# Adding the epsilon of the softmax sum with another VectorE instruction, and moving the embedding scaling into the attention loop

## The reference

```python
scores = scale * q @ k.T + bias           # 2 batches, 8 heads, 768 positions, head_dim 64
scores = where(is_global | is_local, scores, -1e9)
a = exp(scores - max(scores))
a = a / (sum(a) + 1e-9)                   # the 1e-9 is what the change is about
x = (a @ v), rows gathered to [1536, 512]
# first mixture: top-1 of 8 experts by cosine with normalised embeddings
en = emb / (norm(emb) + 1e-6)
x = gate * relu(x[mask] @ w1[e]) @ w2[e]
# second mixture: all 4 experts, weighted by given probabilities
out = sum_e p[:, e] * relu(x @ w1[e]) @ w2[e]
```

## Time and profile before

| | us |
|---|---|
| median of 3 runs | 911.2 |
| lowest, highest | 910.04, 911.38 |
| the profiled execution, whole | 910.04 |
| its span, first to last instruction | 908.2 |

### The profile page before, as it was taken

One profiled execution on the slowest core, in us unless ns is written; L12 is line 12 of the kernel. 1 busy time (PEld: TensorE's weight loads), 2 busy tenths in 40 slices (PEclk: granted clock), 3 DMA queues, 4 the chain that ended last, 5 costly groups with the idle time before them and its releaser, 6 DMA issues.

```text
span 908.2 us, 12900 instructions
## 1 busy us (share of the span) xinstructions
PE 860.9 (95%) x4433; PEld 695.1 (77%) x4434; DVE 300.3 (33%) x776; ACT 221.3 (24%) x476; POOL 288.8 (32%) x162
## 2 busy tenths in 40 slices
PE   7999945999999999999999999999999999999998
PEld 5666623788888788788888888888888888888886
DVE  6777770444444443223121212121212121211212
ACT  4878750033333323311111111111111111111010
POOL 4462613057777778630000650000830001400000
PEclk9999976999999999999999999999999999999999
DMA  6899623146666667620000230000320000001001
GB/s 246 265 315 342 221 78 140 31 124 213 205 204 205 195 220 220 174 94 1 1 0 0 70 116 0 0 0 0 115 71 0 0 0 0 1 0 46 29 17 46
DMA packets 33075, 90.96 MB, mean 100 GB/s; under 512 B 4232, under 2 KB 4616, under 8 KB 33040
## 3 DMA queue, kind: packets, MB, share of 16 engines
q1 hardware_dynamic: 23056, 54.86, 18.1%
q10 hardware_dynamic: 8064, 29.36, 10.6%
q0 software_dynamic: 1920, 6.29, 2.2%
HBM read 72.67 MB, written 17.83 MB: 100 GB/s over the span
## 4 chain that ended last, share of the span: by engine, by line
PE 84%; DMA 8%; DVE 3%; issue 2%; POOL 2%; SPq 1%; ACT 1%; DVEq 0%; ACTq 0%
PE ps L1209 29%; PE ps L1196 29%; PE ps L1153 10%; PE ps L1135 7%; DMA win<-qkv 3%; DMA xg<-x_sorted 3%; PE ps L1008 2%; PE ps L1034 2%; PE ps L1020 2%; POOL x_sorted L473 1%; PE ps L1143 1%; PE ps L1125 1%; PE ps L979 1%; PE ps L1048 1%; ACT arena L528 1%
## 5 line engine op out<-in xcount | busy, mean ns | idle before, releaser
L1209 PE MATMUL ps<-ring,h 128*128 128x512 f32 x1152 | 275.9, 390 | 0.0
L1196 PE MATMUL ps<-ring 128*128 (+1 forms) x864 | 256.4, 389 | 0.0
L278 POOL TENSOR_TENSOR ring<-raw,ring 128x1024 fp32r<-128x1024 f32 x96 | 227.9, 2403 | 84.0 <-ACT ring L273 81.1
L1209 PEld LDWEIGHTS ps<-ring,h 128*128 128x128 f32 x1152 | 215.6, 188 | 44.6
L1196 PEld LDWEIGHTS ps<-ring 128*128 128x128 f32 x864 | 162.1, 188 | 34.0 <-DVE x2b L940 0.2
L947 DVE SCALAR_TENSOR_TENSOR h<-ps,h 128x512 fp32r<-128x512 f32 x96 | 66.3, 691 | 366.3 <-ACT h L597 366.3
L597 ACT ACTIVATE h<-ps 128x512 fp32r<-128x512 f32 x96 | 57.6, 600 | 427.3 <-PE ps L1196 427.3
L273 POOL CAST ring<-raw 128x1024 fp32r<-128x1024 f32 x36 | 38.0, 1055 | 374.8 <-PE ps L1196 320.3
L1196 PE MATMUL ps<-x2b,ring 128*128 (+1 forms) x288 | 112.0, 389 | 0.0
L273 ACT CAST ring<-raw 128x1024 fp32r<-128x1024 f32 x60 | 62.2, 1051 | 176.9 <-PE ps L1153 116.7
L1135 PE MATMUL ps<-ring,xT 128*128 x384 | 91.8, 395 | 0.6 <-DVE xT L900 0.6
(11 more groups left out here) (116 smaller groups left out, 490.2 us busy)
## 6 DMA issues: line engine op xcount, KB each, us to landing
raw<-wts ACTq DMA_DIRECT2D x56, 512.0 KB, 4.2
raw<-wts SPq DMA_DIRECT2D x40, 512.0 KB, 3.8
win<-qkv SPq DMA_DIRECT2D x32, 320.0 KB, 4.1
x_sorted<-ring SPq DMA_DIRECT2D x20, 256.0 KB, 4.9
xg<-x_sorted SPq DMA_DIRECT2D x17, 256.0 KB, 3.4
y_sorted<-yrow SPq DMA_DIRECT2D x16, 256.0 KB, 4.0
win<-qkv SPq DMA_DIRECT2D x8, 384.0 KB, 6.3
result<-xrow SPq DMA_DIRECT2D x12, 256.0 KB, 2.1
```

Of the source, the lines that this page charges most:

```text
L278: nc.gpsimd.tensor_tensor(w_part(u, 1)[:, q * CW:q * CW + CW], raw[:, q, :], w_part(u, 0)[:, q * CW:q * CW + CW].bitcast(F32), ALU.subtrac ...
L1196: ins = nc.tensor.matmul(ps[:, 4 + f % 2, :], w_part(u1, wp)[:, k * F + f * P:k * F + f * P + P], x2T(xp, k)[:, bass.ds(g * 512, 512)], st ...
L1209: ins = nc.tensor.matmul(ps[:, t, :], h2[:, f % 2, hp_, t * P:t * P + P], w_part(u1 + 1, wp)[:, f * DM:f * DM + DM], start=(f == 0 and n = ...
```

## The change

1. `sums` loses its last axis and is [128, 12, 2]. The memset of the constant 1e-9 goes. ScalarE's accumulator writes the same values to the new places.
2. `denominators` is a `tensor_scalar` that adds the immediate 1e-9 to 2 values per partition, where it was a `tensor_reduce` from 4 values to 2. It stands at the same place in the pipeline, 48 times.
3. `scale_embeddings` is no longer called ahead of the bias table. It is run beside the first pair of heads after step 1 (the other branch, which these inputs do not take, calls it at its start).
4. The unused tensor `spare` (160 bytes per partition) goes. With the smaller `sums` all tensors after it lie 256 bytes lower, and `den`, `inv` and `nmax` 96 bytes lower.

```diff
-        sums = sb("sums", [P, DUO, 2, 2])
+        sums = sb("sums", [P, DUO, 2])
...
-        sb("spare", [P, 40])
...
-                                                   accum_out=sums[:, i, hh, 0:1])
+                                                   accum_out=sums[:, i, hh:hh + 1])
...
-            nc.vector.memset(sums[:, :, :, 1], 1e-9)
...
-            scale_embeddings()
...
-                    nc.vector.tensor_reduce(den[:, i % 2, :], sums[:, i, :, :], AX.X, ALU.add).then_inc(denom_ready, 1)
+                    nc.vector.tensor_scalar(den[:, i % 2, :], sums[:, i, :], 1e-9, None, ALU.add).then_inc(denom_ready, 1)
...
-                         {3: keep_embeddings, 6: expert_weights}, {squares: 5})
+                         {1: scale_embeddings, 3: keep_embeddings, 6: expert_weights}, {squares: 5})
```

More of the change, by code:

```diff
@@ L650, in _, with scale_embeddings @@
             dve.wait_ge(bias_built, 1)
+            def scale_embeddings():
+                dve.wait_ge(emb_root, 1)
+                step(nc.vector.tensor_scalar(norm_e[:, 2:3], norm_e[:, 1:2], 1e-6, None, ALU.add))
+                step(nc.vector.reciprocal(norm_e[:, 3:4], norm_e[:, 2:3]))
+                nc.vector.tensor_scalar(embn_t, emb_t, norm_e[:, 3:4], None, ALU.mult).then_inc(emb_scaled, 1)
+                nc.vector.memset(lg[:, :, :, :], 0.0)
+                step(nc.vector.memset(turner[:, :, P:], 0.0))
             def keep_embeddings(idle_times=2):
@@ L750, in _ @@
                                (normalise, 4)],
-                         {3: keep_embeddings, 6: expert_weights}, {squares: 5})
+                         {1: scale_embeddings, 3: keep_embeddings, 6: expert_weights}, {squares: 5})
             with dve.Else():
                 done[0] = before_paths
+                scale_embeddings()
                 keep_embeddings(1)
```

## The result

| | before, us | after, us |
|---|---|---|
| median (4 runs each, same chip) | 911.29 | 922.96 |
| lowest, highest | 910.04, 911.38 | 920.11, 924.50 |
| span of the profiled execution | 908.2 | 920.3 |

A forecast was written before the change was run, and what follows sets the result against it. TensorE was taken to bound attention, with 0.67 us of slack per step. Holds of 3.7 + 3 + 3.8 = 10.5 us on the profiled 910.04 gave 920.5, forecast as 921, range 910.5 to 928.

The forecast's parts named there:

- What bounds the kernel: Attention: TensorE sets the 2.06 us step almost without idle time; VectorE delays up to 0.67 us are hidden.
- Part 1: Embedding scaling moved behind step 1: frees nothing ahead of the bias table and fits a 1.83 us VectorE hole; cost 0.
- the embeddings miss their hole: Rival at attention's start: the multiplication slips, stands until GpSimd's subtraction ends, 1 to 2 us more; inside the forecast's case.
- start: Attention from 12.66 to 26.53 us: denominators held by GpSimd's first four quarters, 3.7 us lost after slack.
- Part 2: Dropped memset and tensors moved by 256 bytes: 0, with 0.5 us to both sides for the addresses.
- Part 3: The 48 new tensor_scalar instructions in attention: each waits for the end of GpSimd's current instruction; 10.5 us in all.
- L732's or L713's: Bounds for the new instruction: never held like the reciprocal, 0 us, or held like the SBUF tensor_scalar; the second was taken.
- middle, eight quarters: Attention's eight single GpSimd quarters: holds partly recovered from TensorE's window waits, 3 us, bounds 1 and 6.
- last four quarters: Attention from 97.75 to 112.35 us: one step per GpSimd quarter, square held again, 3.8 us, bounds 1 and 6.
- Two values take no second port: Rival: the new instruction is never held, like the reciprocal; 911 us, not slower; chance 0.20.
- Held, but hidden: Rival: waits fall into slack and window waits, only attention's start pays; 2 to 5 us, 913 to 916; chance 0.12.
- Faster: Rival: a gain from shorter undisturbed instructions, at most 0.8 us, or an earlier bias table; chance 0.02.

The follow-up runs named there:

- e5: The kernel after with each GpSimd cast and subtraction of attention's quarters made in two instructions of 512 columns: 916.27 us, ratio 1.0012.
- e1: The kernel before with only the embedding scaling moved behind step 1: 910.39 us, ratio 1.0008.
- e3: The kernel after with 256 bytes put back behind nmax, so later tensors lie where they lay before: 922.20 us, ratio 1.0121.
- e10: The kernel before with only 32 bytes more of unused space behind nmax: 927.94 us, ratio 1.0147.
- e11: The kernel before with only 64 bytes more of unused space behind nmax: 930.62 us, ratio 1.0183.
- e4: The kernel after with denominators as two tensor_scalar instructions of one value each, in place of one of two: 912.29 us, ratio 1.0014.
- e6: The kernel after without the denominators stage, the reciprocal reading the two sums in its place, 1e-9 left out: 915.54 us, ratio 0.9991.
- e2: The kernel before with only the new sums and the two-value tensor_scalar, scaling left ahead of the bias table: 923.44 us, ratio 1.0135.

## Why the prediction was right, step by step

**What bounds the kernel.** Right: TensorE sets the pace with little slack, and what is lost in attention reaches the end. (From 28 to 102 us TensorE also waited 1.0 us for VectorE and ScalarE, beside the 3.2 us for windows that I named, and a quarter takes 3.47 us by its own rows, not 3.45; neither enters the sum.) Nothing behind attention makes up for the 10.8 us by which it ends late. The slack of 0.67 us fits e5, where holds of at most 1.25 us in place of 2.29 leave almost nothing of the loss.

**Part 1, the embeddings: 0.** The cost is right (e1: 1.0008), one step of it wrong. I let the multiplication run in 0.43 us beside GpSimd. It slipped past the start of the subtraction, as the rival *the embeddings miss their hole* says: the timeline of VectorE after has

```profile
6.03 0.62 DVE L633 TENSOR_SCALAR xrow<-xrow,nf 128x768 f32<-128x768 f32 x1 [2.12 <-DMA xrow<-consts]
...
13.50 2.49 DVE L645 TENSOR_SCALAR xrow<-xrow,norm_e 8x512 f32<-8x512 f32 x1
```

But the price of that rival, 1 to 2 us, did not come. The held instruction moved VectorE to the end of a subtraction, and the cast L654, which used to be held for 2.22 us, then ran in 0.43. The start summed to 2.88 us where I had 3.7, rival and all. The table starts at 6.03 behind the constants, as predicted.

**Part 2, the addresses: 0 within 0.5.** Right for the 256 bytes (e3), but "nothing in the trace depends on an address" was no ground for a bound. 32 or 64 bytes cost this kernel 13 to 17 us (e10, e11). A trace of one layout can't show what another does, and the bound should have said so.

**Part 3, the hold.** Right in kind: the longest of the line is 2.29 us (2.3 to 2.5 predicted), and its median 170 ns (about 150). The choice between the bounds, L732's or L713's, was the step that carried everything; e4, e5 and e6 bear it out. That a reciprocal is another case than a `tensor_scalar`, though it too has one input and two values, is now shown and no longer argued. The Trainium skill's "Vector Engine (DVE) Microarchitecture Reference" (5.1 Performance modes) lets two elements from SBUF run with both ports. L722's 2290 ns agrees.

The terms:

| term | predicted | measured |
|---|---|---|
| start | 3.7 | 2.9 |
| middle, eight quarters | 3 (1 to 6) | 2.7 |
| a longer wait for a window, then the slow clock | none | 2.7 (0.14 + 1.28 + 1.28) |
| last four quarters | 3.8 (1 to 6) | 2.6 |
| behind attention | 0 | 1.3 |
| sum, against the profiled execution | 10.5 | 12.1 |

The three terms of the hold were each set too high, 10.5 for 8.1 in all. One reason that the rows suggest is that I counted the new waiting and not all of the old that it replaces: L713's 2331 ns, which had left TensorE idle for 0.69 us, is gone, its line now having a mean of 694 ns. In the last stretch the reason is the square: I had it held again, and it came behind GpSimd's last subtraction, which gives 1.9 us back. The steps of 3.4 us came as predicted, though only from the 38th on. What filled the gap I had not in the sum. I had expected the waits for windows only to shrink. Their total does, from 3.2 us to 2.3, but the longest grew from 0.9 to 1.7 us, and the slow clock followed it. The trace narrows down why that window came late: SyncE issued it at 90.29 where it did at 84.77, 5.52 us later and so no later than attention itself, but it took 7.4 us to land in place of 6.2. Why the transfer took longer is open. Of the 1.3 us behind attention, 1.0 lie behind the first scatter (776.6 us to the end for 775.6), which is less than executions of one kernel differ by (920.11 to 924.50); they are open too. So the 921 and the 922.96 agree better than their parts, and that is in part luck: the three terms of the hold were 2.4 us too high in all, and 4.0 us that I had not in the sum came on top.

**The rivals.** *Two values take no second port* fell with the first row of L722. *Held, but hidden* fell as well: 22.9 us of holding left 8.1 us on the path, about a third, and not 2 to 5. *Faster* had no ground. *The embeddings miss their hole* happened and cost nothing that e1 can tell.

## What to carry to other kernels

Before replacing an instruction on one of VectorE's SBUF tensors, look in the trace for the longest duration of the same operation beside GpSimd, not at its median; a count of instructions, or their undisturbed durations, does not show it. If such an instruction can't be avoided, cut it to one value, use another operation, or cut GpSimd's instructions in two: in this kernel each of the three left at most 0.4% of loss (e4, e6, e5), and the last did so without touching the waiting engine. When an experiment adds or removes a small tensor, keep the addresses of all others, or the result may be the layout's.

## What the runs showed of the hardware that I had not expected

- One value against two. A `tensor_scalar` of 128x1 from SBUF to SBUF was not held in 96 cases (156 ns), one of 128x2 up to 2290 ns. A reciprocal of 128x2 was never held (168 ns), a `tensor_tensor` with two SBUF inputs of 128x2 up to 2336 ns, and the reduction from 128x4 of the kernel before never (159 ns).
- The place of tensors in SBUF changes the time of matmuls: 1152 instructions of 128x512 take 390 ns each on the given addresses and 396 and 395 with the tensors 32 and 64 bytes further. The whole kernel is 1.5% and 1.8% slower by it.
- One hold can take the place of another: the multiplication held for 1.52 us left the total as it was (e1, 1.0008). Held for 2.49 us in the kernel after, it left attention 2.88 us late at the 5th `denominators`, where e2 without the move has 3.0.
- A single idle stretch of 1.7 us on TensorE was followed by 3.6 us at a granted clock of 0.55, with 1.00 before it. It cost 1.5 us besides the wait itself. It was seen in one execution; in e2 a wait of 1.1 us at the same step was followed by 1.00.
